# Where the weight tiles begin in a partition, relative to the operand arena

## The chip, the cores and the metric

The kernel runs on one NeuronCore of a Trainium2 chip. The metric is the device time of one execution in microseconds, and lower is better. The kernel before takes 856.04 us (the median of three runs, 855.88 to 856.47).

## The reference

The program computes banded attention and then two feed-forward layers in float32:

```python
scores = scale * q @ k.T + bias        # 4 batches, 8 heads, 576 positions, head size 64
scores = where(0 <= rel < 128, scores, -1e9)
x = softmax(scores) @ v                # to x of 2304 tokens x 512
h = x @ w_in                           # 512 -> 2048
x = (h * sigmoid(1.702 * h)) @ w_out   # 2048 -> 512
h = x @ moe2_w_in
g = where(h >= 1, h, where(h <= -1, 0, (h + 1) ** 2 / 4))
return g @ moe2_w_out
```

## The kernel before

**Attention** fills the first 139 us. Scores are products of 256 columns (`scores`, L1006): a query tile is the stationary operand, the keys move, once as `qk_hi` (the rounded part) and once as `k_lo` (what rounding left). Probabilities are transposed against an identity (`transpose_probs`, L1019), multiplied by the values (`weigh_values`, L1034 and L1040), and the result of a pair of heads is transposed again (L1049, L1054).

**The two layers** fill the rest, and nearly all of it is one line, `multiply` at L1072. Tokens come in three chunks of 768 (two halves of 384). A layer is worked off in two phases (`u` from 0 to 3 in all), each with half of the hidden columns: first three chunks "up" (two duos of products each), then three chunks "down". Products are made by Strassen's scheme: seven operands of the tokens and seven of the weights, `OPS = 7`, instead of eight products of quadrants. Each operand is kept as a rounded part and the remainder (float32r), so one product of two tiles is three matmuls: high by high, high by low, low by high.

Three tensors in SBUF feed L1072:

- `arena`, eight slots of 6,144 bytes per partition with the tokens' operands (high part and low part, 3,072 bytes each, or 6,144 bytes each in two slots). ACT writes the high part (L1330), DVE the low one (L1752).
- `w_first` and `w_rest`, three weight slots each of 14,336 bytes. Weight `w` is in slot `w % 6`: slots 0 to 2 are in `w_first`, 3 to 5 in `w_rest`.

In the up products and in the down products of phases 0 and 1 a weight tile of 128 columns is stationary and 384 columns of the arena move. In the down products of phases 2 and 3 an arena tile of 128 columns is stationary and 256 columns of the weights move:

```python
steps = [(bank, w[:, wh, kt * P:(kt + 1) * P], at[:, xh, kt]) ...          # up: stationary w, moving arena
steps = [(bank, w_op(8 * u + 4 + kt, i)[:, wh, pos * P:(pos + 1) * P], at[:, xh, kt]) ...   # down, u < 2
steps = [(bank[...], at[:, xh, kt, ...], w_op(8 * u + 4 + kt, i)[:, wh]) ...                # down, u >= 2
```

A down product takes its four weights in the order `kt` = 0 to 3, three matmuls (or six) each, so it changes between `w_first` and `w_rest` within the product wherever its four slots lie in both. In phase 0 these are the slots 4, 5, 0, 1, so six matmuls on one tensor follow six on the other. In phase 2 they are 2, 3, 4, 5 (three on `w_first`, nine on `w_rest`), in phase 3 again 4, 5, 0, 1.

The order of all work is written out by hand for each engine. The tensors are laid one behind the other by the helper `sb` in the order of their declarations, each start rounded up to 32 bytes. The attention's tensors are released by `attn_ctx.close()` and `d1s`, `w_rest`, `g`, `ust` and `raw_rest` take their place. The first bytes of a partition belong to a DMA scratch and to four constants, so `w_first` begins at byte 1,152.

Of the kernel before, what the change touches and what calls it, by code (L numbers as in the profile page):

```python
# [20 lines left out]
F32 = mybir.dt.float32  # L21
F32R = mybir.dt.float32r
ALU = mybir.AluOpType
ACT = mybir.ActivationFunctionType

P = 128
# [86 lines left out]
def build(nc, qkT, v_main, v_tail, w_pairs, bias_table, identity, out):  # L113
# [3 lines left out]
    def sb(name, shape, dt, into=ctx):  # L117
        return into.enter_context(nc.sbuf_tensor(name, shape, dt))

    def sem(name):  # L120
        return ctx.enter_context(nc.semaphore(name))

    def f32(ap):
        return ap.bitcast(F32)
# [5 lines left out]
    wd = nc.dram_tensor("wd", (len(STOCK), P, OPS, 2, 2 * P), F32, kind="Internal").ap()  # L130
    zd = nc.dram_tensor("zd", (TOKENS, D_MODEL), F32, kind="Internal").ap()

    w_first = sb("w_first", [P, 3, OPS, 2, 2 * P], F32R)
    arena = sb("arena", [P, ARENA * 4 * HALF], F32R)
    raw_first = sb("raw_first", [P, 3, 4 * HALF], F32)
    wst = sb("wst", [P, 12, 2 * P], F32)
    half = sb("half", [P, 1], F32)

    qk_raw = sb("qk_raw", [P, SPLIT_RING, WIDTH], F32, attn_ctx)
    qk_hi = sb("qk_hi", [P, SPLIT_RING, WIDTH], F32R, attn_ctx)  # L140
# [41 lines left out]
    cleared = sem("cleared")  # L182
# [55 lines left out]
    g_squared = sem("g_squared")  # L238
# [10 lines left out]
    def pair_end(q):  # L249

        return max(m for m, (pair, _) in enumerate(ORDER) if pair == q)
# [5 lines left out]
    def group_of(m):  # L257

        return next(i for i, (_, last) in enumerate(GROUPS) if last >= m)
# [66 lines left out]
    def up_duo(u, c, dd):  # L326
        return u * DUOS + 2 * c + dd
# [10 lines left out]
    def hidden_index(u, c, dd):  # L338
        return (u * CHUNKS + c) * 2 + dd
# [625 lines left out]
    def _(pe):  # L965
# [5 lines left out]
        def first_scores():  # L971

            blocks = ITEMS[FIRST_ORDER[0]]
            for n_pass, k in enumerate((keys(qk_hi, 0), k_lo[:, 0])):
                pe.wait_ge(first_split[0], n_pass + 1)
                for i, (_, blk) in enumerate(blocks):
                    key0, query0 = (blk - 1) * P, QUERIES_AT[0] + blk * P
                    last = nc.tensor.matmul(score_bank[0][:, i * BAND:(i + 1) * BAND], qk_hi[:, 0, query0:query0 + P],
                                            k[:, key0:key0 + BAND], skip_group_check=True,
                                            start=n_pass == 0 and i == 0, stop=n_pass == 1)  # L980
            last.then_inc(scores_ready, 1)
# [243 lines left out]
    def _(act):  # L1225
# [183 lines left out]
        def activate(u, c, dd, tiles=(0, 4)):  # L1409

            D, e = up_duo(u, c, dd), hidden_index(u, c, dd)
            if u < 2:
                act.wait_ge(c22_done, D + 1)
                act.wait_ge(c12_done, D + 1)
                nc.scalar.activation(g[:, e % 2, 1:3], g[:, e % 2, 1:3], ACT.Gelu_apprx_sigmoid).then_inc(g_ready, 1)
            else:
                act.wait_ge(g_clipped, e + 1 - 2 * CHUNKS * 2)
                at = ust[:, tiles[0]:tiles[1]]
                nc.scalar.activation(at, at, ACT.Square, bias=half[:], scale=0.5).then_inc(g_squared, tiles[1] - tiles[0])

        def y_free(engine, u, c):
            wait_past(engine, y_stored, 16 * (u * CHUNKS + c))
# [26 lines left out]
        def up(u, c):  # L1449
# [20 lines left out]
            if c:  # L1470
                activate(u, c - 1, 1)
            elif k == 0:
                round_weights(MADE[2], 1)
                round_weights(MADE[3], 0)
            else:
                round_both(w + (3 if u < 2 else 4))
# [11 lines left out]
            if c < 2:  # L1488
# [7 lines left out]
                if c == 1 and u < 2:  # L1496
                    round_both(UP_STOCK[u][1])
                activate(u, c, 0)
                up_c11(u, c, 1)
                if c == 0 and u < 2:  # L1500
# [5 lines left out]
            else:  # L1506
# [7 lines left out]
                if u >= 2:  # L1514
                    activate(u, c, 0, (0, 2))
# [57 lines left out]
    def _(dve):  # L1573
# [3 lines left out]
        nc.vector.memset(v_sb[TAIL:P, :, 4], 0.0).then_inc(cleared, 1)  # L1577
        for e in range(2):
            nc.vector.memset(f32(qk_hi[:, e::2, ZEROS_AT[e]:ZEROS_AT[e] + TAIL]), 0.0).then_inc(cleared, 1)
        nc.vector.memset(half[:], 0.5).then_inc(cleared, 1)  # L1580

        def round_first():

# [470 lines left out]
```

## Time and profile before

| what | value |
|---|---|
| median of 3 runs | 856.04 us |
| span of the profiled execution, first to last instruction | 854.5 us |
| what lies around the span, by the median | 1.5 us |
| TensorE, share of the span busy | 99% |
| VectorE, ScalarE, GpSimd | 83%, 63%, 14% |
| granted TensorE clock | 1.000 |
| matmuls in all, of them at L1072 | 5,744, 4,536 |

The span is the time between the program's first and last instruction on the core. "Busy" is the union of an engine's instructions, and a matmul's length in the records (336 ns for 384 columns) is much longer than the distance from its start to the start of the next, because matmuls overlap. So here times of the matrix engine are read as distances between starts.

### The profile page before, as it was taken

The numbers are of one execution on the slowest core, as the hardware profiler recorded it, in microseconds if no ns is written. First come the engines' busy times: TensorE is split into PE (matmuls) and PEld (weight loads), VectorE is DVE, ScalarE is ACT, GpSimd is POOL, SyncE is SP. The second block draws the span as 40 slices with busy tenths as digits, with TensorE's granted clock in tenths as the row PEclk, the third lists the DMA queues.
The fourth block names the chain that finished last, engine by engine and source line by source line (L and its number), as shares of the span: only waits on it lengthen the run. The fifth ranks groups of instructions, "written<-read, shape, count | busy, mean of one in ns | idle before, by whom it ended". The sixth has DMA issues, their size and how long they took to land.

```text
span 854.5 us, 15510 instructions
## 1 busy us (share of the span) xinstructions
PE 847.2 (99%) x5744; PEld 843.0 (99%) x5744; DVE 712.3 (83%) x982; ACT 538.6 (63%) x791; POOL 116.3 (14%) x82
## 2 busy tenths in 40 slices
PE   8999999999999999999999999999999999999998
PEld 7999999999999999999999999999999999999998
DVE  7888898786988966868988897989989788889784
ACT  7778786767765546768644456767465567665441
POOL 3788888000000000000000000000000000000000
PEclk9999999999999999999999999999999999999999
DMA  8988661767776337686764772687647643889722
GB/s 198 228 211 216 189 181 67 276 239 279 262 243 238 128 138 271 258 310 239 262 243 177 273 243 103 219 284 260 229 143 278 225 156 124 288 302 331 270 74 75
DMA packets 63257, 186.45 MB, mean 218 GB/s; under 512 B 7504, under 2 KB 14352, under 8 KB 59344
## 3 DMA queue, kind: packets, MB, share of 16 engines
q1 hardware_dynamic: 62896, 185.30, 63.6%
q8 instruction: 47, 0.77, 0.4%
q14 instruction: 26, 0.21, 0.1%
q10 hardware_dynamic: 288, 0.16, 0.1%
HBM read 113.09 MB, written 72.35 MB: 217 GB/s over the span
## 4 chain that ended last, share of the span: by engine, by line
PE 93%; DVE 3%; POOL 1%; DMA 1%; issue 1%; ACT 0%; SPq 0%; DVEq 0%; POOLq 0%
PE ps L1072 81%; PE ps L1040 5%; PE ps L1006 3%; PE ps L1019 3%; DMA raw_first<-yd 1%; POOL qk_hi L892 1%; PE ps L1034 1%; POOL k_lo L889 1%; PE ps L1049 1%; DVE probs L1642 1%; DVE qk_hi L1610 0%; DMA qk_raw<-qkT 0%; DVE arena L1752 0%; DVE qk_hi L1594 0%; ACT probs L1244 0%
## 5 line engine op out<-in xcount | busy, mean ns | idle before, releaser
L1072 PE MATMUL ps<-arena,w_first 128*128 128x384 f32 x1764 | 331.3, 336 | 0.0
L1072 PEld LDWEIGHTS ps<-arena,w_first 128*128 128x128 f32 x1764 | 310.7, 188 | 0.9 <-DVE arena L1752 0.5
L1072 PE MATMUL ps<-arena,w_rest 128*128 128x384 f32 x1260 | 240.4, 336 | 0.3 <-DVE ust L1855 0.3
L1072 PEld LDWEIGHTS ps<-arena,w_rest 128*128 128x128 f32 x1260 | 220.2, 188 | 0.8 <-DVE arena L1752 0.7
L1752 DVE TENSOR_TENSOR arena<-raw_first,arena 128x768 fp32r<-128x768 f32 (+1 forms) x114 | 148.9, 1319 | 77.1 <-ACT arena L1330 77.1
L1330 ACT ACTIVATE arena<-raw_first 128x768 fp32r<-128x768 f32 (+1 forms) x120 | 132.0, 1117 | 45.8 <-DVE raw_first L1711 38.8
L1072 PE MATMUL ps<-w_rest,arena 128*128 128x256 f32 x945 | 132.5, 281 | 0.0
L1072 PEld LDWEIGHTS ps<-w_rest,arena 128*128 128x128 f32 x945 | 121.1, 189 | 0.1
L1072 PE MATMUL ps<-w_first,arena 128*128 128x256 f32 x567 | 88.0, 282 | 0.0
L1752 DVE TENSOR_TENSOR arena<-raw_rest,arena 128x1536 fp32r<-128x1536 f32 (+1 forms) x48 | 71.4, 1487 | 8.6 <-ACT arena L1330 8.4
L1072 PEld LDWEIGHTS ps<-w_first,arena 128*128 128x128 f32 x567 | 76.0, 189 | 0.0
L1330 ACT ACTIVATE arena<-raw_rest 128x1536 fp32r<-128x1536 f32 (+1 forms) x48 | 60.9, 1268 | 23.0 <-PE ps L1072 21.0
L1376 ACT ACTIVATE d1s<-ps 128x384 f32<-128x384 f32 (+2 forms) x72 | 35.3, 490 | 40.9 <-PE ps L1072 40.9
L1244 ACT ACTIVATE probs<-probs,neg_max 128x256 f32<-128x256 f32 (+1 forms) x128 | 54.1, 472 | 6.5 <-DVE neg_max L1642 6.5
L1040 PE MATMUL ps<-v_sb,probs_t 128*128 128x65 f32 x448 | 57.1, 268 | 0.5 <-DVE heads_out L1655 0.5
L1040 PEld LDWEIGHTS ps<-v_sb,probs_t 128*128 128x128 f32 x448 | 55.3, 191 | 1.1 <-issue 0.9
L1642 DVE CUSTOM_DVE_ANT_0 probs<-ps,bias_sb 128x256 f32<-128x256 f32 (+1 forms) x128 | 44.6, 387 | 12.9 <-PE ps L1006 8.6
L1367 ACT ACTIVATE ps<-ps 128x384 f32<-128x384 f32 (+2 forms) x72 | 34.2, 476 | 30.1 <-PE ps L1072 28.9
L1674 DVE TENSOR_TENSOR wst<-wst 128x256 f32<-128x256 f32 (+1 forms) x90 | 48.5, 539 | 2.8
L1284 ACT ACTIVATE probs_t<-ps 128x512 f32<-128x512 f32 x64 | 37.8, 591 | 18.4 <-PE ps L1019 18.1
L1006 PE MATMUL ps<-qk_hi 128*128 128x256 f32 x158 | 47.6, 324 | 1.4 <-DVE qk_hi L1594 0.5
L892 POOL TENSOR_TENSOR qk_hi<-qk_raw,qk_hi 64x576 fp32r<-64x576 f32 x28 | 45.2, 1613 | 2.2
(125 smaller groups left out, 970.5 us busy)
## 6 DMA issues: line engine op xcount, KB each, us to landing
gd<-g SPq DMA_DIRECT2D x24, 1536.0 KB, 6.1
raw_rest<-gd SPq DMA_DIRECT2D x32, 768.0 KB, 5.1
wst<-w_pairs SPq DMA_DIRECT2D x32, 512.0 KB, 5.7
raw_first<-gd SPq DMA_DIRECT2D x16, 768.0 KB, 5.9
yd<-ust SPq DMA_DIRECT2D x6, 1536.0 KB, 6.3
qk_raw<-qkT SPq DMA_DIRECT2D x30, 288.0 KB, 4.1
wd<-ust SPq DMA_DIRECT2D x4, 1536.0 KB, 8.4
raw_first<-yd SPq DMA_DIRECT2D x4, 1536.0 KB, 7.7
```

Source lines behind the costliest of these rows:

```text
L892: nc.gpsimd.tensor_tensor(all_queries(qk_hi, head, LOWER), all_queries(qk_raw, head, UPPER), f32(all_queries(qk_hi, head, UPPER)), ALU.sub ...
L1006: last = nc.tensor.matmul(place, queries, k[:, key0:key0 + BAND], start=n_pass == 0 and (d > 0 or i == 0), stop=n_pass == 1 and (d > 0 or ...
L1040: last = nc.tensor.matmul(o_slot(2 * blk + e), probs_t[:, gi % 2, col:col + P], v_sb[:, h + e, max(blk - 1, 0) + piece], start=piece == 0, ...
L1072: last = nc.tensor.matmul(to, stationary, moving, start=start and n == 0, stop=n == len(steps) - 1, skip_group_check=True)
L1244: last = nc.scalar.activation(at, at, ACT.Exp, bias=neg_max[:, col:col + 1], scale=-1.0)
L1284: nc.scalar.activation(probs_t[:, gi % 2], pt_bank[gi % 2], ACT.Copy).then_inc(pt_copied[gi % 2], 1)
L1330: nc.scalar.activation(operand(k, i)[:, 0], source(k, i), ACT.Copy).then_inc(hi_made, 1)
L1367: nc.scalar.activation(b_bank(D, pos), a_bank(D, pos), ACT.Copy).then_inc(seeded_b, 1)
L1376: nc.scalar.activation(d1(D, pos), d_bank(D, pos), ACT.Copy).then_inc(d_copied, 1)
L1642: last = nc.vector.tensor_tensor_reduce(out=to[:, 0:width], in0=bank[:, i * BAND:i * BAND + width], in1=bias_sb[:, h + e, BAND - width:BAN ...
L1674: nc.vector.tensor_tensor(to, a, b, ALU.subtract).then_inc(w_added, 1)
L1752: nc.vector.tensor_tensor(at[:, 1], source(k, i), f32(at[:, 0]), ALU.subtract).then_inc(lo_made, 1)
```

## The change

Two pads of 64 bytes per partition are declared, one ahead of `w_first` and one ahead of `arena`, and `half` (one float, the bias of an activation) is given a full 64 bytes:

```diff
+    sb("before_w_first", [P, 16], F32)
     w_first = sb("w_first", [P, 3, OPS, 2, 2 * P], F32R)
+    sb("before_arena", [P, 16], F32)
     arena = sb("arena", [P, ARENA * 4 * HALF], F32R)
     raw_first = sb("raw_first", [P, 3, 4 * HALF], F32)
     wst = sb("wst", [P, 12, 2 * P], F32)
-    half = sb("half", [P, 1], F32)
+    half_line = sb("half", [P, 16], F32)
+    half = half_line[:, 0:1]
```

and `half[:]` becomes `half` where it is set and used. No instruction is added, removed or moved. What changes is where tensors begin in a partition; worked out from the declarations, as the remainder of the first byte by 128:

| tensor | before | after | is, for TensorE |
|---|---|---|---|
| `w_first` | 0 | 64 | stationary or moving |
| `arena` | 0 | 0 | moving or stationary |
| `w_rest` | 32 | 64 | stationary or moving |
| `raw_first`, `wst`, `half` | 0 | 0 | |
| `d1s`, `g`, `ust`, `raw_rest`, `qk_raw` | 32 | 64 | |
| `qk_hi`, `k_lo` | 32 | 64 | stationary and moving |
| `ident`, `probs`, `probs_tail` | 64 | 96 | moving, stationary |
| `probs_t`, `heads_out` | 0 | 32 | stationary |
| `v_sb` | 32 | 64 | moving, rows of 260 bytes |

Slots and tiles of weights and arena are multiples of 128 bytes, so every operand of L1072 has the remainder of its tensor.

## Rows read from the trace of the kernel before

**Rows 1.** The page: busy share of each engine, granted clock, chain by line.

```profile
PE 847.2 (99%) x5744; PEld 843.0 (99%) x5744; DVE 712.3 (83%) x982; ACT 538.6 (63%) x791; POOL 116.3 (14%) x82
...
PEclk9999999999999999999999999999999999999999
...
PE ps L1072 81%; PE ps L1040 5%; PE ps L1006 3%; PE ps L1019 3%; DMA raw_first<-yd 1%; POOL qk_hi L892 1%; PE ps L1034 1%; POOL k_lo L889 1%; PE ps L1049 1%; DVE probs L1642 1%; DVE qk_hi L1610 0%; DMA qk_raw<-qkT 0%; DVE arena L1752 0%; DVE qk_hi L1594 0%; ACT probs L1244 0%
```

**Rows 2.** Groups by form, PE: names, shapes, count, busy us, mean ns, idle us.

```profile
L1072 PE MATMUL ps<-arena,w_first 128*128 128x384 f32 x1764 | 331.3, 336 | 0.0
L1072 PE MATMUL ps<-arena,w_rest 128*128 128x384 f32 x1260 | 240.4, 336 | 0.3 <-DVE ust L1855 0.3
L1072 PE MATMUL ps<-w_rest,arena 128*128 128x256 f32 x945 | 132.5, 281 | 0.0
L1072 PE MATMUL ps<-w_first,arena 128*128 128x256 f32 x567 | 88.0, 282 | 0.0
L1040 PE MATMUL ps<-v_sb,probs_t 128*128 128x65 f32 x448 | 57.1, 268 | 0.5 <-DVE heads_out L1655 0.5
L1006 PE MATMUL ps<-qk_hi 128*128 128x256 f32 x158 | 47.6, 324 | 1.4 <-DVE qk_hi L1594 0.5 <-DVE qk_hi L1602 0.4 <-POOL qk_hi L892 0.3
...
L1019 PE MATMUL ps<-ident,probs 128*128 128x128 f32 x224 | 35.5, 275 | 0.4 <-ACT probs L1244 0.2
```

**Rows 3.** Timeline of PE, 384 columns, one weight tensor: start us, length us, what.

```profile
171.80 16.46 PE L1072 MATMUL ps<-arena,w_first 128*128 128x384 f32 x94
...
362.45 16.80 PE L1072 MATMUL ps<-arena,w_rest 128*128 128x384 f32 x96
```

**Rows 4.** Timeline of PE, 384 columns, the weight tensors by turns.

```profile
241.53 1.21 PE L1072 MATMUL ps<-arena,w_rest 128*128 128x384 f32 x6
242.58 1.23 PE L1072 MATMUL ps<-arena,w_first 128*128 128x384 f32 x6
243.64 1.21 PE L1072 MATMUL ps<-arena,w_rest 128*128 128x384 f32 x6
...
313.16 1.21 PE L1072 MATMUL ps<-arena,w_rest 128*128 128x384 f32 x6
```

**Rows 5.** Timeline of PE, 256 columns, phases 2 and 3 down.

```profile
603.84 0.51 PE L1072 MATMUL ps<-w_first,arena 128*128 128x256 f32 x3
604.19 1.22 PE L1072 MATMUL ps<-w_rest,arena 128*128 128x256 f32 x9
605.25 0.53 PE L1072 MATMUL ps<-w_first,arena 128*128 128x256 f32 x3
605.61 1.23 PE L1072 MATMUL ps<-w_rest,arena 128*128 128x256 f32 x9
...
663.48 0.51 PE L1072 MATMUL ps<-w_first,arena 128*128 128x256 f32 x3
...
838.48 0.88 PE L1072 MATMUL ps<-w_rest,arena 128*128 128x256 f32 x6
...
844.19 0.88 PE L1072 MATMUL ps<-w_rest,arena 128*128 128x256 f32 x6
```

**Rows 6.** Timeline of PE, keep-warm matmuls, both operands in `arena`.

```profile
6.67 2.08 PE L969 MATMUL ps<-arena 128*128 128x256 f32 x16
```

**Rows 7.** Timeline of PE in attention.

```profile
101.55 1.00 PE L1040 MATMUL ps<-v_sb,probs_t 128*128 128x65 f32 x8
102.39 0.61 PE L1019 MATMUL ps<-ident,probs 128*128 128x128 f32 x4
...
105.18 0.60 PE L1049 MATMUL ps<-ident,heads_out 128*128 128x128 f32 x4
```

**Rows 8.** Groups by form, DVE and ACT, same shape at remainder 0 and 32.

```profile
L1752 DVE TENSOR_TENSOR arena<-raw_first,arena 128x1536 fp32r<-128x1536 f32 x52 | 90.9, 1754 | 25.7 <-ACT arena L1330 25.7
L1752 DVE TENSOR_TENSOR arena<-raw_rest,arena 128x1536 fp32r<-128x1536 f32 x32 | 56.1, 1754 | 7.1 <-ACT arena L1330 7.0
...
L1330 ACT ACTIVATE arena<-raw_first 128x1536 fp32r<-128x1536 f32 x52 | 76.6, 1481 | 28.4 <-DVE raw_first L1711 27.6 <-DVE raw_first L1706 0.7
...
L1330 ACT ACTIVATE arena<-raw_rest 128x1536 fp32r<-128x1536 f32 x32 | 47.4, 1482 | 21.0 <-PE ps L1072 21.0
```

More of the change, by code:

```diff
@@ L1418, in activate @@
                 at = ust[:, tiles[0]:tiles[1]]
-                nc.scalar.activation(at, at, ACT.Square, bias=half[:], scale=0.5).then_inc(g_squared, tiles[1] - tiles[0])
+                nc.scalar.activation(at, at, ACT.Square, bias=half, scale=0.5).then_inc(g_squared, tiles[1] - tiles[0])
         def y_free(engine, u, c):
@@ L1579, in _ @@
             nc.vector.memset(f32(qk_hi[:, e::2, ZEROS_AT[e]:ZEROS_AT[e] + TAIL]), 0.0).then_inc(cleared, 1)
-        nc.vector.memset(half[:], 0.5).then_inc(cleared, 1)
+        nc.vector.memset(half, 0.5).then_inc(cleared, 1)
         def round_first():
```

## The prediction, made before the changed kernel ran

> **What bounds the kernel now.** I read the page first. TensorE is busy 99% of the span, its clock is granted in full (2.4 GHz, the upper level) in all 40 slices, and the chain that ended last lies 81% on L1072 [rows 1]. The groups by form say what L1072 is: 1764 matmuls of 384 columns with weights from `w_first`, 1260 with weights from `w_rest`, and 945 + 567 = 1512 of 256 columns in which the weights move; none of the groups waits for more than 0.3 us [rows 2]. DVE (83%) and ACT (63%) are behind the matrix engine, not ahead of it. So the time is 4536 times the distance between two starts, and a change that moves no instruction can matter only if it changes that distance. The timeline gives it: first start to last end of a run, less one length, over the number less one.
>
> - 94 matmuls on `w_first` alone: (16.46 - 0.336) / 93 = 173.4 ns. 96 on `w_rest` alone: (16.80 - 0.336) / 95 = 173.3 ns [rows 3]. The two tensors stand at the remainders 0 and 32, and both give the same distance.
> - In phase 0 down six on one alternate with six on the other. From the `w_rest` run at 241.53 to the one at 313.16 there are 34 such turns, 408 matmuls: 71.63 us / 408 = 175.6 ns [rows 4]. At 173.3 ns they would take 70.71 us, so each turn costs 0.92 us / 34 = 27 ns more. The rows show where: from the start of a `w_rest` run to that of the next `w_first` run it is 1.05 us (242.58 - 241.53), from `w_first` to `w_rest` 1.06 us (243.64 - 242.58), against 6 x 0.1733 = 1.04.
>
> 384 columns at 2.4 GHz are 160 ns. So 13.3 ns of the 173.3 are something else, at either remainder.
>
> **The change, part by part.**
>
> *Turns at 384 columns.* With both weight tensors at 64 there is no change of remainder within a run. In the timeline a `w_rest` group of 384 columns is followed by a `w_first` group 129 times. If it is the changed remainder that costs, 129 x 27 ns = 3.5 us go [rows 4]. All of it is on the path, since TensorE's distances are the path. This is the term I trust most. Its bounds: 0, if something other than the remainder makes the turn dear; 3.5.
>
> *The steady distance at 384 columns.* It is 173.3 ns at 0 and at 32 [rows 3]; nothing in the trace has weights at 64 against a moving tensor at 0. I take 173.3, since two different remainders agree to 0.1 ns. Its ends, from below and above, are the rivals.
>
> *256 columns.* Phase 2 down: from the `w_first` run at 603.84 to the one at 663.48, 42 turns of 12 matmuls, 59.64 us / 504 = 118.3 ns. Phase 3 down: (844.19 - 838.48) / 48 = 119.0 ns. So the mean is 118.6. Nine on `w_rest` in a row take 1.06 us, 117.8 ns each [rows 5]. The keep-warm matmuls, with both operands in `arena` at the same remainder, settle at (2.08 - 0.28) / 15 = 120.0 ns [rows 6]. So here the remainder shows, by 2 ns. At 64 it could be either: 1512 x (120.0 - 118.6) = +2.1 us at one end, 1512 x (117.8 - 118.6) = -1.2 us at the other. I take 0, which is between them.
>
> *Attention.* The score matmuls keep equal remainders on both sides (32 and 32, then 64 and 64). For the transposes and the value products the stationary tiles move: `probs_t` and `heads_out` from 0 to 32, `probs` from 64 to 96. Today the transposes of `heads_out` at 0 go at (0.60 - 0.27) / 3 = 110 ns. Those of `probs` at 64 take 0.61 for four, 113 ns, of which the first after a value product holds the difference; the value products take (1.00 - 0.27) / 7 = 104 ns [rows 7]. No row shows 32 or 96 for these. The largest difference between steady runs that a row shows for a remainder is 120.0 - 117.8 = 2.2 ns [rows 5, 6]. The 448 value products and 224 transposes of the rows, with some 180 more of their kinds, at 2.2 ns are 1.9 us either way [rows 2]. I take 0, since 0 and 64 hardly differ.
>
> *DVE, ACT and the transfers.* `raw_rest` and `raw_first` stand at 32 and 0 today, and the same shape takes 1754 and 1754 ns on DVE, 1482 and 1481 ns on ACT [rows 8]. No price, and what little there was would be behind TensorE. DMAs start and land by the same waits as before, and none of them is on the path between two matmuls more than 1% of the span [rows 1].
>
> *The sum.* -3.5 + 0 + 0 + 0 + 0 = -3.5 us, of a profiled span of 854.5 us: about 851.0. By the median of the runs, 856.04, which is the span and 1.5 us around it, the forecast is 852.5 us. The bounds within this case: -3.5 - 1.2 - 1.9 = -6.6 us (849.4), and 0 + 2.1 + 1.9 = +4.0 us (860.0), though not all at once.
>
> **What speaks against any effect.** The turn costs 27 ns in the rows and 34 turns repeat it [rows 4]. The Trainium skill ("TensorE: Matmul & The Clock Gate", Part 2: What happens when you issue a matmul) says that the array reads its moving operand and its weights through two read ports of their own, so that the load of the next weights takes nothing from the running matmul. By that rule no distance would depend on where the two tensors stand against each other, and the time would stay at 856.0 us. This trace does not agree with it to the nanosecond, for there are 13.3 ns over the columns and 27 ns per turn; but the trace can't say whether a turn is dear through the remainder or through the distance of the two tensors, which lie 129,056 bytes apart and will go on doing so. That is the first rival.
>
> **Rivals.**
>
> 1. *The change doesn't do what it says to the distances.* The 27 ns belong to leaving one region for another, 129 times in 384 columns, whatever the remainder. For it: going from `w_first` to `w_rest` costs about nothing, so the cost isn't symmetric, as a mere difference of remainders might be. Against it: at 256 columns the same change of region costs next to nothing in sum (118.3 ns on average over whole turns, [rows 5]). The time would be 856.0 us. Chance 0.16.
>
> 2. *Slower: the state at 64 is the bad one.* After a return to `w_first` six matmuls take 1.06 instead of 1.04 us, and the one before takes its share, so for some four matmuls the distance is about 173.3 + 27 / 4 = 180 ns. If with weights at 64 against an arena at 0 the two streams never fall back into step, that becomes the steady distance: 3024 x 6.8 ns = 20.6 us, less the 3.5 of the turns, 873 us. It decides the sign from where 3024 x d exceeds 3.5 us, that is, from a steady distance of 174.5 ns. For it: 13.3 ns over the columns show that the streams do meet, and the sum has no row at 64. Against it: 0 and 32 both settle at 173.3. Chance 0.13.
>
> 3. *Much faster: the streams no longer meet.* If 64 is just the place at which the load of the next weights and the moving stream keep out of each other's way, up to the whole 13.3 ns at 384 columns and 118.6 - 106.7 = 11.9 ns at 256 columns go: 40 + 18 = 58 us, 798 us. For it: 256 columns already show runs at 117.8 as well as at 120.0, so a remainder can save something [rows 5, 6]. Against it: moving the weights by 32 changed the steady 173.3 not at all, so the 13.3 ns look like a fixed part of each matmul. Chance 0.09; a small part of it (an eighth, 5 to 8 us) would end at 848 to 851.
>
> **How the numbers follow.** The main case, in which the turns go and all else stays near where it is, has 0.62; its own range is 849.4 to 858, since its corner at 860.0 needs every bound at once. The rivals have 0.16, 0.13 and 0.09. The range must hold eight in ten: the main case and the first rival are 0.78, and the ends at 848.5 and 858.5 leave out only the far corners of the main case and take in the near parts of the other two. A measurement of this kernel tells about 0.2% (1.7 us) from no change. The main case gains more than that unless the 256-column matmuls settle at 120 or attention loses: about three quarters of it, 0.47, and rival 3 with 0.09, give 0.56 for faster. Within 0.2% are rival 1 (0.16) and some 0.12 of the main case, 0.28. Slower are rival 2 (0.13) and 0.03 of the main case, 0.16.
>
> **What would show it.** In the profile after, the long runs on one weight tensor at 173.3 ns [rows 3], phase 0 down at 173.3 instead of 175.6 ns, that is 70.7 instead of 71.6 us for its 408 matmuls [rows 4]. If those still cost 27 ns a turn, rival 1 holds. If the long runs move, up or down, rival 2 or 3 holds, and the sum is 3024 times the difference. The 256-column runs decide the rest: 118.6 ns now, between 117.8 and 120.0 I expect. TensorE's busy share stays at 99%, and DVE and ACT groups keep their means. The prediction is wrong if the time falls outside 848.5 to 858.5 us, and its reason is wrong if the time falls but the turns are as dear as before.

## The result, and the profile after

The changed kernel takes 852.61 us (median of five runs, 852.53 to 853.5), against 855.95 us for the kernel before on the same chip. The ratio is 0.9961, with an interval of 0.9951 to 0.9972: 0.4% faster, by 3.3 us. The profiled execution has a span of 850.8 us, against 854.5 before. The forecast of 852.5 us is met to 0.1 us, and the rest of this document shows that it was met by two errors that nearly cancel.

The page of the changed kernel, the lines that answer to [rows 1]:

```profile
PE 843.7 (99%) x5744; PEld 839.7 (99%) x5744; DVE 711.4 (84%) x982; ACT 538.5 (63%) x791; POOL 116.4 (14%) x82
...
PEclk9999999999999999999999999999999999999999
```

Nothing but TensorE moved: 3.5 us less busy time for the same 5,744 matmuls, at a granted clock of 0.999 against 1.000, while DVE, ACT and GpSimd kept theirs to 1 us. `multiply` is line 1075 now. Its four groups, as in [rows 2] (busy us, mean ns of one, idle us ahead):

```profile
L1075 PE MATMUL ps<-arena,w_first 128*128 128x384 f32 x1764 | 328.6, 336 | 0.0
L1075 PE MATMUL ps<-arena,w_rest 128*128 128x384 f32 x1260 | 241.4, 336 | 0.0
L1075 PE MATMUL ps<-w_rest,arena 128*128 128x256 f32 x945 | 131.9, 280 | 0.6 <-DVE g L1858 0.6
L1075 PE MATMUL ps<-w_first,arena 128*128 128x256 f32 x567 | 85.8, 278 | 0.0
```

This already contradicts the forecast's sum. The first group gained (331.3 to 328.6), but the second **lost** (240.4 to 241.4), and the 256-column groups, on which I had put nothing, gained 2.2 and 0.6. The timeline says why. Two long runs on one weight tensor, and the alternation of phase 0 down (start us, length us), as in [rows 3, 4]:

```profile
171.11 16.80 PE L1075 MATMUL ps<-arena,w_first 128*128 128x384 f32 x96
...
238.99 1.21 PE L1075 MATMUL ps<-arena,w_rest 128*128 128x384 f32 x6
240.04 1.21 PE L1075 MATMUL ps<-arena,w_first 128*128 128x384 f32 x6
...
310.16 1.21 PE L1075 MATMUL ps<-arena,w_rest 128*128 128x384 f32 x6
...
361.52 16.93 PE L1075 MATMUL ps<-arena,w_rest 128*128 128x384 f32 x96
```

- On `w_first` the distance is (16.80 - 0.336) / 95 = 173.3 ns, as forecast. On `w_rest` it is (16.93 - 0.336) / 95 = 174.7 ns, where it was 173.3. Both tensors now have the same remainder by 128, and they do not behave alike.
- Phase 0 down: 71.17 us for 34 turns, 174.4 ns a matmul, against 175.6 before. The plain mean of 173.3 and 174.7 would be 174.0, so a turn still costs 0.4 x 12 = 5 ns instead of 27.

The 256 columns, as in [rows 5]:

```profile
601.90 0.51 PE L1075 MATMUL ps<-w_first,arena 128*128 128x256 f32 x3
602.25 1.22 PE L1075 MATMUL ps<-w_rest,arena 128*128 128x256 f32 x9
...
661.26 0.51 PE L1075 MATMUL ps<-w_first,arena 128*128 128x256 f32 x3
...
788.82 0.85 PE L1075 MATMUL ps<-w_first,arena 128*128 128x256 f32 x6
790.27 0.92 PE L1075 MATMUL ps<-w_rest,arena 128*128 128x256 f32 x6 [0.61 <-DVE g L1858]
...
834.25 0.85 PE L1075 MATMUL ps<-w_first,arena 128*128 128x256 f32 x6
...
839.82 0.85 PE L1075 MATMUL ps<-w_first,arena 128*128 128x256 f32 x6
```

Phase 2: (661.26 - 601.90) / 504 = 117.8 ns, before 118.3. Phase 3: (839.82 - 834.25) / 48 = 116.0 ns, before 119.0. The forecast's window was 117.8 to 120.0, so this is under it. And at 790.27 there is a wait of 0.61 us that before did not have: the earlier matmuls arrive before VectorE's addition into `g` (L1858), so a part of the gain is handed to VectorE.

Summing the distances between starts over all of the trace gives the account in full. A wait lies between the start before it and the start behind it, so it is counted with the matmul before it, here one on `w_first`:

| matmuls at L1075 | before, us | after, us | difference |
|---|---|---|---|
| 384 columns, `w_first` | 309.47 | 306.90 | -2.57 |
| 384 columns, `w_rest` | 219.63 | 220.39 | +0.76 |
| 256 columns, `w_first`, with the new wait | 67.35 | 65.99 | -1.36 |
| 256 columns, `w_rest` | 112.00 | 111.56 | -0.44 |
| together | 708.45 | 704.84 | -3.61 |

384 columns give -1.8 us where -3.5 was forecast, 256 columns -1.8 us where 0 was. Without the wait the 256 columns on `w_first` alone would have given some 2.1 us.

### The profile page after: what moved, and what is told of

Read it like the earlier page. It is cut to its first block, busy times and chain, and to the rows that moved or that the text cites. A ratio compares the mean times of both kernels' runs of the same rounds, so it can differ in the third digit from the quotient of the medians.

```text
span 850.8 us, 15510 instructions
## 1 busy us (share of the span) xinstructions
PE 843.7 (99%) x5744; PEld 839.7 (99%) x5744; DVE 711.4 (84%) x982; ACT 538.5 (63%) x791; POOL 116.4 (14%) x82
## 4 chain that ended last, share of the span: by engine, by line
PE 92%; DVE 5%; POOL 1%; issue 1%; ACT 0%; DVEq 0%; POOLq 0%
PE ps L1075 79%; PE ps L1043 4%; PE ps L1009 3%; PE ps L1022 3%; DVE arena L1755 1%; PE ps L972 1%; POOL qk_hi L895 1%; PE ps L1037 1%; POOL k_lo L892 1%; PE ps L1052 1%; DVE probs L1645 1%; DVE qk_hi L1613 0%; DVE raw_first L1714 0%; DVE g L1787 0%; DVE raw_first L1709 0%
## 5 line engine op out<-in xcount | busy, mean ns | idle before, releaser
L1075 PE MATMUL ps<-arena,w_first 128*128 128x384 f32 x1764 | 328.6, 336 | 0.0
L1075 PEld LDWEIGHTS ps<-arena,w_first 128*128 128x128 f32 x1764 | 307.2, 188 | 0.9 <-DVE arena L1755 0.3
L1075 PE MATMUL ps<-arena,w_rest 128*128 128x384 f32 x1260 | 241.4, 336 | 0.0
L1075 PEld LDWEIGHTS ps<-arena,w_rest 128*128 128x128 f32 x1260 | 221.8, 188 | 0.6 <-issue 0.3
L1075 PE MATMUL ps<-w_rest,arena 128*128 128x256 f32 x945 | 131.9, 280 | 0.6 <-DVE g L1858 0.6
L1075 PEld LDWEIGHTS ps<-w_rest,arena 128*128 128x128 f32 x945 | 120.0, 188 | 0.8 <-issue 0.8
L1075 PE MATMUL ps<-w_first,arena 128*128 128x256 f32 x567 | 85.8, 278 | 0.0
L1075 PEld LDWEIGHTS ps<-w_first,arena 128*128 128x128 f32 x567 | 74.8, 188 | 0.0
L1645 DVE CUSTOM_DVE_ANT_0 probs<-ps,bias_sb 128x256 f32<-128x256 f32 (+1 forms) x128 | 44.6, 387 | 13.3 <-PE ps L1009 8.7
```

Source lines behind the costliest of these rows:

```text
L1075: last = nc.tensor.matmul(to, stationary, moving, start=start and n == 0, stop=n == len(steps) - 1, skip_group_check=True)
L1645: last = nc.vector.tensor_tensor_reduce(out=to[:, 0:width], in0=bank[:, i * BAND:i * BAND + width], in1=bias_sb[:, h + e, BAND - width:BAN ...
```

## The experiments

The question is what the distance depends on, since "the remainder by 128" can't explain 173.3 on one tensor and 174.7 on the other. Worked out from the declarations, the starts in bytes are:

| | `w_first` | `arena` | `w_rest` | weights minus arena, by 256: `w_first`, `w_rest` |
|---|---|---|---|---|
| before | 1,152 | 44,160 | 130,208 | 0, +32 |
| after | 1,216 | 44,288 | 130,368 | -64, +64 |

Below, "offset" is this: where the weights begin minus where the arena begins, taken by 256; -64 is the same as 192. **Theory A:** the offset by 256 bytes sets the distance. **Theory B:** the period is 128 bytes, and something else tells the two tensors apart. **Theory C:** the region or the absolute place of a tensor matters.

### A map of the offset, in a kernel of its own

Sixteen weight tiles `w_a` to `w_p` begin 0, 32, ... 480 bytes behind the arena's start by 512; 90 matmuls run on each, first with the weights stationary and 384 columns of the arena moving, then with 256 columns of the weights moving:

```python
arena = sb("arena", [P, 6 * 384], F32R)                           # 18 * 512 bytes
tiles = [sb(f"w_{n}", [P, 6 * P + 8], F32R) for n in NAMES]       # 6 * 512 + 32 bytes each
...
nc.tensor.matmul(ps[:, 0, 0:384], t[...P columns...], arena[...384 columns...], start=True, stop=True)
nc.tensor.matmul(ps[:, 1, 0:256], arena[...P columns...], t[...256 columns...], start=True, stop=True)
```

> This kernel leaves out all of the computation: it only runs matmuls on constant data and stores zeros. One arena tile and 16 weight tiles w_a to w_p that begin 0, 32, 64, ... 480 bytes behind it by the remainder of 512; 90 matmuls of 384 columns with the weights stationary on each, then 90 of 256 columns with the weights moving on each, high/high, high/low, low/high as in the kernel. Theory A (the distance between starts follows from the offset of the weights against the arena, period 256 or 512 bytes): 384 columns at 173.3 ns for offsets 0, 32 and 448 (-64), 174.5 ns for 64; 256 columns at 120 ns for 0, about 118 for 32 and 64, 115 for 448; w_i to w_p differ from w_a to w_h if the period is 512 and repeat them if it is 256. Theory B (period 128, as the change's wording has it): w_a, w_e, w_i and w_m agree in both shapes, and w_c agrees with w_o. Theory C (region of the memory, not the offset): all 16 tiles agree within 0.5 ns, or drift from w_a to w_p without a repeat.

Rows of its timeline (start us, length us; the distance is the length less one matmul's, over 89):

```profile
49.18 15.88 PE L44 MATMUL ps<-arena,w_c 128*128 128x384 f32 x90
...
80.49 16.00 PE L44 MATMUL ps<-arena,w_e 128*128 128x384 f32 x90
96.33 16.07 PE L44 MATMUL ps<-arena,w_f 128*128 128x384 f32 x90
112.24 15.76 PE L44 MATMUL ps<-arena,w_g 128*128 128x384 f32 x90
...
143.74 15.76 PE L44 MATMUL ps<-arena,w_i 128*128 128x384 f32 x90
...
174.94 15.88 PE L44 MATMUL ps<-arena,w_k 128*128 128x384 f32 x90
...
206.26 16.00 PE L44 MATMUL ps<-arena,w_m 128*128 128x384 f32 x90
...
269.50 10.95 PE L53 MATMUL ps<-w_a,arena 128*128 128x256 f32 x90
...
312.29 10.85 PE L53 MATMUL ps<-w_e,arena 128*128 128x256 f32 x90
...
333.53 10.39 PE L53 MATMUL ps<-w_g,arena 128*128 128x256 f32 x90
...
418.43 10.39 PE L53 MATMUL ps<-w_o,arena 128*128 128x256 f32 x90
```

Read them by pairs. `w_c` (64) and `w_k` (320 = 256 + 64) both take 15.88 us, `w_e` (128) and `w_m` (384) both 16.00, `w_g` and `w_o` both 10.39: all repeat after 256 bytes (`w_a`, the first to run, is disturbed by the start at 384 columns). `w_e` (128) is not `w_i` (256), 16.00 against 15.76, so 128 bytes are not a period. The steady distances, in the middle of each run (whole runs at 256 columns, with the change-over, have means up to 0.4 ns off):

| offset | 0 | 32 | 64 | 96 | 128 | 160 | 192 | 224 |
|---|---|---|---|---|---|---|---|---|
| 384 columns, ns | 173.3 | 173.3 | 174.6 | 173.3 | 176.0 | 176.7 | 173.3 | 176.7 |
| 256 columns, ns | 120.0 | 117.8 | 117.8 | 120.0 | 118.7 | 117.4 | 113.3 | 118.3 |

The changed kernel's two long runs are in it: 173.3 at 192, 174.6 at 64. Theory B falls, and C has nothing left to explain, since neighbours and far tiles repeat exactly. The table has one limit: each offset was measured behind one predecessor only, and tiles 256 bytes apart had the same one.

### Each half of the change alone

The arena's offset to `w_first` is set by the two pads, that to `w_rest` by `half`. So the change has two halves. Only the second (against the changed kernel):

```diff
-    sb("before_w_first", [P, 16], F32)
-    sb("before_arena", [P, 16], F32)
```

> Only the 64 bytes of half: w_first and arena stay at 0, w_rest begins 64 bytes behind (offset +64 against the arena). Theory A: runs of 384 columns on w_rest at 174.5 ns as after the change, runs on w_first at 173.3; 256 columns on w_rest at 118.0, on w_first near 119 to 120. With the turns as dear as before (27 ns) the time is 856 + 1260 x 0.9 ns = 857 us; with turns at 5 ns or less 854 us. Theory C (each region has its own distance, and the turn is dear by the region): 856 us, like the kernel before.

Measured: 857.68 us (857.51 to 858.24), ratio 1.0019 (1.001 to 1.0028), **slower** than before by 1.65 us. Offsets 0 and +64 alternate in phase 0 down:

```profile
245.72 1.22 PE L1073 MATMUL ps<-arena,w_rest 128*128 128x384 f32 x6
246.78 1.21 PE L1073 MATMUL ps<-arena,w_first 128*128 128x384 f32 x6
...
249.92 1.22 PE L1073 MATMUL ps<-arena,w_rest 128*128 128x384 f32 x6
```

4.20 us for 24 matmuls, 175.0 ns, nearly the 175.6 of before. But the turns are not what is dear here. The long run on `w_rest` is:

```profile
362.45 17.12 PE L1073 MATMUL ps<-arena,w_rest 128*128 128x384 f32 x96
```

(17.12 - 0.336) / 95 = 176.7 ns, where the changed kernel and the map have 174.6 for the same offset of +64; five of the six long runs on `w_rest` in this trace stand there, and the long runs on `w_first` at 173.3. The mean of 173.3 and 176.7 is 175.0, so the turns cost nothing. Theory A misses here, although its 857 us came close: 174.5 ns with dear turns was expected, and 176.7 ns with free turns was found. The offset alone does not set the distance at 384 columns either. In the changed kernel these matmuls follow runs at -64, here runs at 0; that the way in decides between 174.6 and 176.7 is made likely by the 256 columns below, but no run tests it at this width.

Only the first half:

```diff
-    half_line = sb("half", [P, 16], F32)
+    half_line = sb("half", [P, 1], F32)
```

> Only the two pads: w_first 64 bytes ahead of the arena by the remainder (-64), w_rest 32 behind it as before. Theory A: w_first at 173.3 ns (384) and 115 ns (256) as after the change, w_rest at 173.3 and 117.8 as before; 256 columns give 567 x 3.6 ns = 2.0 us, 384 columns on w_rest 1.1 us more than the change gave: 851.5 us if the turns are cheap, 854 us if they cost 27 ns. Theory that both must stand at the same remainder for the turns to be cheap: turns at 27 ns, 854 us or more.

Measured: 850.84 us (850.77 to 850.91), ratio 0.994 (0.9926 to 0.9953). The pads alone are worth 5.2 us, and the full change is 1.8 us slower than its own first half. Offsets -64 and +32 alternate here:

```profile
246.30 1.20 PE L1075 MATMUL ps<-arena,w_first 128*128 128x384 f32 x6
...
250.46 1.20 PE L1075 MATMUL ps<-arena,w_first 128*128 128x384 f32 x6
```

4.16 us for 24 matmuls is 173.3 ns: the turns are free, though the two tensors still differ in remainder (64 and 32 by 128). So what made a turn dear before was not a change of offset as such: between +32 and 0 it costs 27 ns, between +64 and 0 and between -64 and +32 nothing.

### Both at -64

No offset of the map is below -64 (192) in either row. `half` with 448 bytes puts `w_rest` there too:

```diff
-    half_line = sb("half", [P, 16], F32)
+    half_line = sb("half", [P, 112], F32)
```

> half takes 448 bytes, so w_rest too begins 64 bytes ahead of the arena by the remainder of 512 (-64), like w_first; by the remainder of 128 nothing differs from the change. Theory A: w_rest goes from 174.5 to 173.3 ns (1260 x 1.2 = 1.5 us) and from 118.0 to 115.2 ns (945 x 2.8 = 2.6 us): 848.5 us. Theories B and C: 852.6 us as after the change, since the remainder by 128 and the regions are the same.

Measured: 851.87 us (850.01 to 851.97), ratio 0.9947 (0.9935 to 0.996). Some 0.7 us faster than the change, with intervals that overlap, 3.4 us short of the 848.5 expected, and not faster than the pads alone. The 384 columns are as expected, at 173.4 ns on both tensors. The 256 columns are not:

```profile
600.70 0.52 PE L1075 MATMUL ps<-w_first,arena 128*128 128x256 f32 x3
...
603.53 0.52 PE L1075 MATMUL ps<-w_first,arena 128*128 128x256 f32 x3
```

2.83 us for 24 matmuls, 117.9 ns, where the map has 113.3 for this offset. 1512 matmuls at 4.5 ns are 6.8 us that did not come. The second miss for theory A as I had it, now at 256 columns.

### A finer map, and the order of the runs

A second small kernel has offsets between (16 to 240 by 32), other widths, and at offset 192 (`w_under`) 256-column runs behind different predecessors.

> Leaves out all of the computation, like the first probe. (1) Offsets of 16, 48, 80, ... 240 bytes (w_a to w_h) between the ones measured: theory A, period 256 and nothing finer than 32 bytes: each lies between its neighbours (384 columns 173.3 to 176.7 ns, 256 columns 113.3 to 120). If the best offset is a narrow point, 176 and 208 are as dear as their far neighbours. (2) Offset 0 with 256, 320, 448 and 512 columns moving: if the 13.3 ns over the columns are a fixed part of a matmul, 120.0, 146.7, 200.0, 226.7 ns; if they grow with the columns, the last is 160 x 4/3 + 17.8 = 231 ns. (3) w_under stands at 192 (-64). 256 columns on it right after 384 columns on it, after offset 0, and after each of w_a to w_h: if the third kernel's 117.9 ns instead of 113.3 comes from the state in which the run begins, some of these runs settle at 113.3 and others at about 118 and stay there; if it comes from the tiles of the kernel, all settle at 113.3.

The steady distances, again in the middle of the runs:

| offset | 16 | 48 | 80 | 112 | 144 | 176 | 208 | 240 |
|---|---|---|---|---|---|---|---|---|
| 384 columns, ns | 173.3 | 173.3 | 176.0 | 177.8 | 177.3 | 173.3 | 175.6 | 173.3 |
| 256 columns, ns | 116.7 | 118.3 | 120.0 | 113.3 | 118.7 | 119.3 | 119.2 | 117.2 |

At offset 0, 256, 320, 384, 448 and 512 columns take 120.0, 146.7, 173.3, 202.7 and 226.7 ns: 13.3 ns over the columns' own time at 2.4 GHz, the level that is granted in this stretch, and 16 at 448. What explains the miss at 256 columns are these four rows (384 columns at 192, 256 at 192, 256 at 0, 256 at 192 again):

```profile
218.08 15.77 PE L48 MATMUL ps<-arena,w_under 128*128 128x384 f32 x90
233.69 10.76 PE L57 MATMUL ps<-w_under,arena 128*128 128x256 f32 x90
244.28 10.96 PE L57 MATMUL ps<-w_zero,arena 128*128 128x256 f32 x90
255.07 10.38 PE L57 MATMUL ps<-w_under,arena 128*128 128x256 f32 x90
```

The same 90 matmuls on the same bytes take 10.76 us behind the 384-column run and 10.38 us behind a run at offset 0: 117.8 and 113.3 ns. Both hold to the end of the 90, once the first few are through. The later runs at 192 in this trace agree: behind 256 columns at 16 and at 48 they are in the upper state, behind those at 80 to 240 in the lower. So 256 columns at 192 have **two stable states**, and the way in decides. In the kernel with both at -64 they come from 384 columns at -64, and stay in the dearer one.

### The whole layout 64 bytes lower

```diff
-    sb("before_w_first", [P, 16], F32)
```

> The change without the pad ahead of w_first: everything lies 64 bytes lower, w_first at 0 and the arena at 64 by the remainder of 128, the offsets against each other as in the change (-64 and +64). Theory A (only the offset counts): 852.6 us, w_first at 173.5 and 115.2 ns, w_rest at 174.6 and 118.1. If the absolute place counts (the arena at a multiple of 128): the distances change, and the time is the one before, 856, or more.

Measured: 852.31 us (852.01 to 853.4), ratio 0.996 (0.9948 to 0.9973), the same as the change, 0.9961. With the arena at a remainder of 64 by 128 and the weights at 0 all offsets are as in the change, and so is the time. The absolute place that the change speaks of has no effect at this shift; the rest of theory C falls. Its profiled run, at 853.4 us the slowest of the five, has 384 columns as in the change (173.6 and 174.5 ns), but the 256 columns on `w_first` at 116.4 ns instead of 115.2: the mixture of states can differ at the same offsets.

### Both at 0, and at 128

Both pairs have weights and arena at a remainder of 0 by 128; by 256 they stand at 0 and 0, and at -128 and +128, which is the same offset. Against the changed kernel:

```diff
-    sb("before_w_first", [P, 16], F32)
-    sb("before_arena", [P, 16], F32)
-    half_line = sb("half", [P, 16], F32)
+    half_line = sb("half", [P, 128], F32)
```

> Weights and arena all at one remainder (offset 0 for both weight tensors; half takes 512 bytes). Theory A: 384 columns at 173.3 ns throughout with no cost at a turn, 256 columns at 120.0 ns, the dearest of the first probe. Against the kernel with the first pads alone (850.8): 1512 x (120.0 - 116.7) = +5.0 us, 855.8 us, though the turns (3.5 us) are gone. If cheap turns are the whole of the gain, 852.5 us.

```diff
-    sb("before_w_first", [P, 16], F32)
-    sb("before_arena", [P, 16], F32)
+    sb("before_arena", [P, 32], F32)
-    half_line = sb("half", [P, 16], F32)
+    half_line = sb("half", [P, 32], F32)
```

> w_first 128 bytes ahead of the arena, w_rest 128 behind: by the remainder of 128 both offsets are 0, by that of 256 both are 128. Theory A with period 256: 384 columns at 176.05 ns (3024 x 2.7 = 8.2 us more than 173.3), 256 columns at 118.7: 850.8 + 8.2 + 1512 x 2.0 ns = 862.0 us. Theory B (period 128): the same as with both at 0, 855.8 us or what that run gives.

Measured: 854.95 us (854.68 to 855.48), ratio 0.9988 (0.9979 to 0.9997) for both at 0; 860.03 us (859.45 to 860.93), ratio 1.0048 (1.0035 to 1.0061) for both at 128. The turns at 384 columns, first of both at 0, then of both at 128:

```profile
239.91 1.20 PE L1073 MATMUL ps<-arena,w_first 128*128 128x384 f32 x6
...
248.23 1.20 PE L1073 MATMUL ps<-arena,w_first 128*128 128x384 f32 x6
```

```profile
241.01 1.22 PE L1074 MATMUL ps<-arena,w_first 128*128 128x384 f32 x6
...
249.45 1.22 PE L1074 MATMUL ps<-arena,w_first 128*128 128x384 f32 x6
```

8.32 us for 48 matmuls, 173.3 ns, against 8.44 us, 175.8 ns. This is the whole kernel, not the small one, and it tells A from B: same remainders by 128, 5.1 us apart, in the direction of the map and near its size (173.3 and 176.0; 862.0 us was expected for both at 128). With both at 0 there is no dear turn at all, and the tensors lie as far apart as ever to within 480 bytes, so the forecast's first rival falls here.

### What moves the 256 columns from one state to the other

In a third small kernel a run of 384 columns at 192 is followed by `n` matmuls with both operands in the arena (offset 0), then by 90 of 256 columns at 192:

```python
columns_384(w_under)
for _ in range(n):                                            # the kick
    nc.tensor.matmul(ps[:, 2, 0:width], arena[:, 0:P], arena[:, 384:384 + width], start=True, stop=True)
columns_256(w_under)
```

> Leaves out all of the computation. Offset 192 (-64) throughout: 90 matmuls of 384 columns, then a kick of n matmuls with both operands in the arena (offset 0; 256 columns wide for n = 0, 1, 2, 3, 4, 6, 9, 12, then 128 columns and 512 columns wide for n = 1, 2, 3, 6), then 90 matmuls of 256 columns. If the lower state (113.3 ns) and the upper one (117.75) are both stable and only the entry decides, n = 0 gives 117.75 as before and some n gives 113.3 for the whole run of 90, the fewer the better. If the lower state needs a long stay at offset 0, no small n changes anything.

Its timeline, without a kick, with three of 256 columns, and with three of 128:

```profile
45.48 10.76 PE L57 MATMUL ps<-w_under,arena 128*128 128x256 f32 x90
...
124.11 0.53 PE L63 MATMUL ps<-arena 128*128 128x256 f32 x3
124.48 10.77 PE L57 MATMUL ps<-w_under,arena 128*128 128x256 f32 x90
...
310.47 0.45 PE L63 MATMUL ps<-arena 128*128 128x128 f32 x3
310.75 10.44 PE L57 MATMUL ps<-w_under,arena 128*128 128x256 f32 x90
```

| kick | the 90 behind it at 113.3 ns | at 117.8 ns |
|---|---|---|
| none | | x |
| 256 columns | 1, 6, 9, 12 matmuls | 2, 3, 4 |
| 128 columns | 2, 3, 6 | 1 |
| 512 columns | 1, 3, 6 | 2 |

All five kicks of six matmuls or more led to the lower state, the shorter ones only at some counts, and no rule for those comes out of it. For the kernel I took three of 128 columns: 0.28 us from their start to the next run's, and two and six of them work as well.

### The best of it in the kernel

Both at -64, and three short matmuls ahead of the first product of the down part in phases 2 and 3. They write the bank that the product itself then starts anew:

```diff
-    half_line = sb("half", [P, 16], F32)
+    half_line = sb("half", [P, 112], F32)
...
             wait_past(pe, c21_out, 2 * (D - 1) + n)
+            if not up and u >= 2 and c == 0 and n == 0:
+                at = operand(k, A11)
+                for _ in range(3):
+                    nc.tensor.matmul(a_bank(D, pos)[:, 0:128], at[:, 0, 0, 0:P], at[:, 1, 0, 0:128], start=True, stop=True)
             multiply(u, up, k, D, P1, pos, a_bank(D, pos), True).then_inc(p1_done, 1)
```

> The kernel with both weight tensors at -64, and three matmuls of 128 columns with both operands in the arena ahead of the first down product of phases 2 and 3 (their result is overwritten). If the state at the entry decides, the 1512 matmuls of 256 columns go at 113.3 to 114 ns instead of 117.8: 1512 x 4.2 = 6.3 us less, 0.8 us more for the kicks, and some of the gain may turn into waits for DVE: 847 us. If the state is lost again at every duo (waits, order of the tiles), 852 to 853 us.

Measured: 847.23 us (846.93 to 848.89), ratio 0.99 (0.9887 to 0.9914).

```profile
581.13 0.44 PE L1109 MATMUL ps<-arena 128*128 128x128 f32 x3
...
600.52 0.50 PE L1075 MATMUL ps<-w_first,arena 128*128 128x256 f32 x3
600.87 1.18 PE L1075 MATMUL ps<-w_rest,arena 128*128 128x256 f32 x9
...
603.25 0.50 PE L1075 MATMUL ps<-w_first,arena 128*128 128x256 f32 x3
```

2.73 us for 24 matmuls, 113.7 ns, where the same kernel without the kick has 2.83 us. Over the whole trace the 256 columns stand at 113.5 ns, on both tensors. 1512 x 4.4 = 6.6 us should come back; 4.6 do (851.87 to 847.23). Twice 0.3 us are the kicks, and VectorE takes the next part:

```profile
L1075 PE MATMUL ps<-w_rest,arena 128*128 128x256 f32 x945 | 127.8, 276 | 1.0 <-DVE g L1862 1.0
```

The wait for the addition into `g` was 0.2 us without the kick and is 1.0 us now: the bound begins to move.

The last run is the same with six matmuls of 256 columns as the kick:

```diff
-                for _ in range(3):
-                    nc.tensor.matmul(a_bank(D, pos)[:, 0:128], at[:, 0, 0, 0:P], at[:, 1, 0, 0:128], start=True, stop=True)
+                for _ in range(6):
+                    nc.tensor.matmul(a_bank(D, pos)[:, 0:256], at[:, 0, 0, 0:P], at[:, 1, 0, 0:256], start=True, stop=True)
```

> The same with six kicks of 256 columns: 1.4 us for them. Where the short kick misses the lower state and this one reaches it, this one is at 847.5 us and the other at 852.5; where both reach it, they differ by 0.7 us; where neither does, both are slower than the kernel without them (851.9).

Measured: 848.02 us (847.77 to 849.96), ratio 0.9916 (0.9902 to 0.993), with the 256 columns at 113.4 ns. The state is the same. The 0.8 us between the two kernels are what the longer kicks should cost, but their runs overlap, so that much is not shown.

### Whether the distances explain the times

Mean distances of the four kinds (without those that hold a wait), their difference to before times the counts 1764, 1260, 567 and 945, and what was measured against the kernel before, run beside it:

| kernel (offsets) | 384 `w_first` | 384 `w_rest` | 256 `w_first` | 256 `w_rest` | worked out, us | measured, us |
|---|---|---|---|---|---|---|
| before (0, +32) | 175.0 | 173.8 | 118.9 | 118.4 | | |
| the change (-64, +64) | 173.5 | 174.6 | 115.2 | 118.0 | -4.1 | -3.3 |
| second half alone (0, +64) | 173.65 | 176.3 | 121.3 | 118.2 | +1.9 | +1.65 |
| first half alone (-64, +32) | 173.34 | 173.36 | 115.5 | 117.5 | -6.3 | -5.2 |
| the layout 64 bytes lower (-64, +64) | 173.6 | 174.5 | 116.4 | 118.1 | -3.4 | -2.55 (its profiled run) |
| both at -64 | 173.37 | 173.38 | 117.8 | 117.9 | -4.5 | -4.2 |
| both at 0 | 173.4 | 173.4 | 119.98 | 119.98 | -1.2 | -1.0 |
| both at 128 | 175.85 | 175.87 | 118.7 | 118.75 | +4.3 | +4.1 |

The order is kept throughout. Where the worked-out gain is large, the measured one is 0.3 to 1.1 us smaller; the waits on VectorE (0.6 us in the change and in its first half) are part of that.

## Why the prediction came out right

- **What bounds the kernel: right.** The time moves with the sum of the distances at L1072; the table above ties seven kernels to it.
- **Turns at 384 columns, -3.5 us, "the term I trust most": the size holds, the reason does not.** The turns went from 27 to 5 ns. But it was not the differing remainder that made them dear. -64 and +32 differ too, and there the turns cost nothing. Dear was the alternation of +32 and 0 (27 ns a turn); +64 and 0 differ as well, and with the second half alone there is no cost at a turn, only a dearer steady distance on `w_rest`. By the sums over the traces, 384 columns take 529.10 us before and 525.70 with both at -64, so the dear turns were worth 3.4 us.
- **The steady distance at 384 columns, "I take 173.3, since two different remainders agree to 0.1 ns": this step failed.** Two points that agree are no law. At +64 the distance is 174.6 in the changed kernel, and 384 columns take 527.29 us there instead of the 525.70: 1.6 us are given back, where 0 was put. `w_first` escaped it only because it stands at -64, which the table of remainders by 128 can't tell from +64. Part of the step that failed is thus the choice of 128 as the modulus, taken over from the change without a row for it. The starts were known from the declarations, the 256 bytes were not: the rows of before hold only the offsets 0 and +32, which say nothing of a period.
- **256 columns, 0 (from -1.2 to +2.1): the second step that failed.** It was -1.8 us, outside the bounds, because I bounded it by the states seen (117.8 and 120.0), and a third one was to be had. In phase 3 down the distances on `w_first` at -64 lie at 114.2 ns in the mean, most of them from 113 to 116, near the lower of its two states, while `w_rest` stays at 117.7; together that is the 116.0.
- **Attention, DVE, ACT, transfers at 0: right.** The first matmul of L1072 starts 0.2 us earlier than before; the large groups of DVE and ACT, and of TensorE in attention, keep their means to 3 ns. That nothing waits was not: the addition into `g` became late, 0.6 us.
- **Rival 1 (no effect) is refuted** by both at 0: the same regions, the same alternation, no dear turn. (The 129,056 bytes between the two tensors do not quite stay either: they are 129,152 after the change.) The Trainium skill ("TensorE: Matmul & The Clock Gate", Part 2: What happens when you issue a matmul) gives the moving operand and the weights a read port each. No run here shows the ports. What the prediction inferred from them, that no distance depends on where the two tensors stand, does not hold: the distance moves between 173.3 and 177.8 ns at 384 columns, and between 113.3 and 120.0 ns at 256, with the offset by 256 bytes.
- **Rival 2 (slower) was partly true.** Its deciding value, 174.5 ns for all 3024, is what `w_rest` reached (174.6), but only 1260 matmuls had it. The second half of the change alone is this rival come true, with 176.7 ns on `w_rest` and 857.68 us, and both at 128 is the larger form, at 860.03 us (175.9 ns throughout), far from the 873 I had worked out.
- **Rival 3 (streams no longer meet):** its small form, 848 to 851 us, was there to be had with the first half alone (850.84), and the kick goes a little beyond it (847.23). No offset came below 173.3 ns at 384 columns, so the 13.3 ns look like a fixed part at this width, as I had put against it; that is not shown. At 256 columns half of it goes (113.3 against 106.7 of columns).

So where the forecast had -3.5 us and nothing else, the trace has -3.4 (turns) + 1.6 (384 columns at +64) - 1.8 (256 columns) = -3.6 us. The size of the turns was earned, by a reason that does not hold; that the rest came to nearly nothing was luck.

What stays open: why the period is 256 bytes, and what the two streams meet at. Why 256 columns at -64 have two steady states, and what rule picks one behind a short kick. Why 384 columns at +64 run at 174.6 ns in the changed kernel and at 176.7 with its second half alone. Some runs lie about 2 us from the others of their kernel (850.01 us against 851.7 to 852.0 with both at -64, 849.9 against 847.8 to 848.0 with the long kick); a state that comes out otherwise would be of that size, but no trace shows it. Nothing here looked into attention's operands, nor at offsets between -64 and +32 in the full kernel.

## What to carry to other kernels

Where TensorE runs back to back, measure the distance between starts for each pair of tensors, and write down where both operands begin by 256 bytes **against each other**; pads of 64 and 128 bytes moved this kernel from 0.6% faster to 0.5% slower. Split a change of layout into its tensors before judging it: here one half alone gained 5.2 us and the other alone lost 1.7, and the sum looked like a modest success. The halves are not independent: `w_rest` at +64 cost 384 columns more without the pads (176.7 ns) than with them (174.6). And when a steady distance in the full kernel differs from that of an isolated loop at the same offset, suspect the state it came in with, not only the bytes.

## What the runs showed that I had not expected

- In the map the distance repeats exactly after 256 bytes of offset (both shapes), and it does not rise or fall evenly with the offset: at 384 columns 173.3 at 96 and 192, but 177.8 at 112 and 176.7 at 160 and 224.
- The best offset depends on the shape: 112 is the dearest of sixteen offsets at 384 columns (177.8 ns) and, with 192, the cheapest at 256 (113.3). Both tables hold for the predecessor that each run had.
- Two steady states for identical instructions on identical bytes, 4% apart (113.3 and 117.8 ns), each holding to the end of 90 matmuls; three matmuls of 128 columns, 0.28 us, lead from the upper to the lower, and with it 4.6 us of the full kernel go. At 384 columns the offset +64 too has two distances, 174.6 and 176.7 ns, each steady over 84 to 96 matmuls.
- At offset 0, matmuls of this type come 13.3 ns later than their columns need at 2.4 GHz, whether 256, 320, 384 or 512 columns wide (16 at 448).
